# A token-mixing and two-layer network kernel: the first tokens split earlier, two weight units finished later, values loaded in longer runs

## The chip, the cores and the metric

The kernel runs on one core of a Trainium2 chip. The metric is the device time of one execution in microseconds; three executions of the kernel before were timed, and one more was recorded by the profiler. TensorE (PE) multiplies matrices, VectorE (DVE), ScalarE (ACT) and GpSimd (POOL) do elementwise work, SyncE (SP) issues most DMAs and POOL some.

## The reference

Three stages follow each other, on 8 batches of 576 tokens with 512 channels (8 heads of 64).

```python
def _attn_ref(q, k, v):
    q_s = exp(q - max(q, axis=-1)); q_s = q_s / (sum(q_s, axis=-1) + 1e-09)
    k_s = exp(k - max(k, axis=2));  k_s = k_s / (sum(k_s, axis=2) + 1e-09)
    kv = einsum('bhsd,bhse->bhde', k_s, v)
    return einsum('bhsd,bhde->bhse', q_s, kv)

def _moe_ref(x, w_tok1, w_tok2, w_ch1, w_ch2):       # w_ch1 512x1536
    h = maximum(x.T(per batch) @ w_tok1, 0.0) @ w_tok2
    u = x + h.T(per batch)
    return u + maximum(u @ w_ch1, 0.0) @ w_ch2

def _moe2_ref(x, g_ln, w_ch1, w_ch2):                # w_ch1 512x2048
    xn = (x - mean) / sqrt(var + 1e-06) * g_ln
    return x + maximum(xn @ w_ch1, 0.0) @ w_ch2
```

## The kernel before

**Attention and token mixing** run over the 8 batches, one `step(i, later)` each on every engine (`batches`). SP loads for the next batch keys, queries, values (`load_k`, `load_q`, `load_v`, L289) and transposed keys (`load_kT`), and stores the result u to DRAM. Every value product on PE (`product_kv`, L1155) multiplies the exponentials of the keys with a tile `vt` that has, for each group of 128 channels, 128 columns of values and one column of ones, whose product is the denominator. `vt` holds 5 token chunks (four of 128 rows, one of 64); one DMA per chunk fills four pieces of 128 floats (512 bytes) in each row. PE waits for all of them (`v_in`). The query side is a chain: maximum on DVE, subtraction on POOL, exponential on ACT, sum and normalisation on DVE, rounding to f32r on ACT (`hi_q`), the remainder on POOL (`lo_q`, L464), whose last part (for the 64-row chunk) is q_hi<-qt and is needed by the product at L1187.

**Precision.** Every product is made of three f32r products: high by high, high by low, low by high (`three`, L1131 to L1133). So each operand is split into a hi part (a cast on ACT) and a lo part (a subtraction on DVE or POOL).

**The two network stages** (B and C) run over tokens in passes of 924 tokens (two halves of 462; the last of a stage 912), five passes a stage. A product of 2x2 blocks is made of seven products of sums of blocks, with the sums formed on the fly. For each pass there are three (B) or four (C) mixing calls (`c.j >= 0`), each with seven products p = 0 to 6, one entry of the weight ring each, and then one finishing call with seven products of several entries (21 in B). An entry is 512 KB in DRAM, loaded by SP into a ring of four (`load_entry`), and it gives PE twelve matmuls. The ring's load n waits until PE is done with entry n - 4.

- `hi_x(pos, p)` (ACT, L566), `lo_x(pos, p)` (DVE, L834) and `sum_x(pos, i)` (DVE, L816 to L828) make the seven split operands of a pass from `xn`. For pass 0 they stand in the last batch's step and behind it: hi_x 0 and 1 in the step, 2 and 3 behind `hi_unit(6)`, 4 to 6 behind the takes of call 0.
- `take(c, p)` (ACT L650, DVE L950) moves a product from PSUM; PE's product p waits for the take of p - 2. `relu(c, p)` is L656.
- `load_x(1, c)` on SP (L328) loads the next pass; its first waits for all seven x_lo of pass 0, and stands in SP's program between ring loads.

**Weight units.** The combined, split weights of the seven products are prepared in the kernel itself, in 28 units (0 to 11 for B, 12 to 27 for C), and stored to a scratch in DRAM from which the ring reads. A unit is: two loads into `w_op` (`load_unit`, L416, L417, POOL's queue), four sums on POOL (`sum_unit`, L423 to L428), the hi part on ACT (`hi_unit`, L550), the lo part in two pieces (`lo_unit`: L434 on POOL or L841 on DVE, signal `wp_lo`), and a store of 1,792 KB (`store_unit`, L447, POOL's queue). `w_op` and `w_out` have two places; load n waits for lo n - 2. Units 0 to 7 are made beside the batches with lo on POOL; units 8 on have hi and lo at positions of the entry order (`HI_AT`), ACT's hi behind the entry's take, DVE's two halves one and two products later. The finishing call's first entries need units: its entry e (e21 + e in the count of ring entries from 0) needs units up to 7 + 2e stored, so e21 needs 0 to 7, e22 up to 9, e23 up to 11.

All orders are written out by hand; each engine runs its program in order and waits on semaphores.

Of the kernel before, what the change touches and what calls it, by code (L numbers as in the profile page):

```python
# [8 lines left out]
def mixer_kernel(nc, q, k, kT, v, w_tok1, w_tok2, w1b, w2b, g_ln, w1c, w2c, out):  # L9
    fp32, f32r = mybir.dt.float32, mybir.dt.float32r  # L10
# [17 lines left out]
    U_DVE, U_ACT = NC // 2, 2 * NC - NC // 2  # L28
    CONSTS = 10


# [21 lines left out]
    for pos in range(NX):  # L53
        stage, sg = "BC"[pos // NSG], pos % NSG
        for j in range(G1S[stage] + 1):
# [8 lines left out]

    UNITS_A = NB
    HI_AT = {e: UNITS_A + i for i, e in enumerate((2, 5, 8, 12, 27, 36))}
    HI_AT.update({(s + 1) * ENTRIES["B"] + e: UNITS_A + 6 + 5 * s + i
                  for s in range(3) for i, e in enumerate((0, 6, 11, 27, 36))})
# [43 lines left out]
    with ctx:  # L112
# [19 lines left out]
        with ExitStack() as u:  # L132
# [4 lines left out]
            with ExitStack() as a:  # L137
                kt = sb("kt", [P, NC, S], fp32, a)
                vt = sb("vt", [P, NT, NC, P + 1], fp32, a)
                ke = sb("ke", [P, NT, C], fp32, a)  # L140
# [134 lines left out]
        def _(sp):  # L275
# [10 lines left out]
            def load_v(b):  # L286
                wait(sp, kv_done, b)
                for t, rows in ST:
                    sp.dma_start(vt[0:rows, t, :, 0:P], v[b, t * P:t * P + rows, :].rearrange("p (c e) -> p c e", c=NC))\  # L289
                      .then_inc(v_in, 16)  # L290

# [113 lines left out]
        def _(pool):  # L405
# [70 lines left out]
            nc.gpsimd.memset(ke[tail, NT - 1, :], 0.0).then_inc(consts_made, 1)  # L476
            nc.gpsimd.memset(vt[tail, NT - 1, :, 0:P], 0.0).then_inc(consts_made, 1)
            pool.wait_ge(consts_made, CONSTS - 1)
# [9 lines left out]
            def step(i, later):  # L488
# [15 lines left out]
                if later:  # L504
                    lo_q(i + 1)
                lo_unit(i - 1)
                store_unit(i - 1)

            batches(step)
            load_unit(NB)  # L510
            sum_unit(NB - 1)
            lo_unit(NB - 1)
            store_unit(NB - 1)
            for n in range(NB, U0["C"] + UNITS["C"]):
                sum_unit(n)
                if n + 1 < U0["C"] + UNITS["C"]:
                    load_unit(n + 1)
                store_unit(n)


        @block.scalar
        def _(act):
# [49 lines left out]
            def step(i, later):  # L572
# [14 lines left out]
                else:  # L587
# [5 lines left out]
                    if later:  # L593
                        exp_k(i + 1, ST[0:1])
                    else:
                        hi_x(0, 0)
                    hi_qT(i, ST[4:])
                    act.wait_ge(g_done, 2 * i + 2)
# [10 lines left out]
                for c in range(NC):  # L609
# [6 lines left out]
                    if later:  # L616
# [6 lines left out]
                        if c >= 1:  # L623
                            hi_q(i + 1, ST[c - 1:c])
                    if later == 0 and c == 0:
                        hi_x(0, 1)
                if later:
# [64 lines left out]

            hi_unit(NB - 2)
            for p in (2, 3):
                hi_x(0, p)
            hi_unit(NB - 1)
            for c in CALLS:
                if c.j >= 0:
                    last = c.j == G1S[c.stage] - 1
                    for p in range(7):  # L700
                        if p in (0, 1, 2, 6):
                            take(c, p)
                        if c.index == 0 and p < 3:
                            hi_x(0, 4 + p)
                        if p == 4:
# [29 lines left out]
        def _(dve):  # L735
# [45 lines left out]
            def norm_kv(b):  # L781
# [3 lines left out]
                wait(dve, krec_made, b)  # L785
                halves = [bank[4][:, 0:2 * (P + 1)].rearrange("p (c e) -> p c e", c=2),
                          bank[1][:, 0:2 * (P + 1)].rearrange("p (c e) -> p c e", c=2)]
                for n, x in enumerate(halves):
                    nc.vector.tensor_scalar(k_den[:, 2 * n:2 * n + 2], x[:, :, P], EPS_SUM, None, ALU.add)\
                      .then_inc(kden_made, 1)  # L790
# [53 lines left out]
            def step(i, later):  # L844
# [12 lines left out]
                else:  # L857
# [15 lines left out]
                    if later:  # L873
                        sub_k(i + 1, ST[1:3])
                        max_q(i + 1, ST[2:3])
                for m in range(ND):
                    dve.wait_ge(rhi_made, ND * i + m + 1)
                    nc.vector.scalar_tensor_tensor(out=r_lo[:, m, :], in0=bank[(7, 2)[m]][:, :], scalar=0.0,
                                                   in1=r_hi[:, m, :], op0=ALU.max, op1=ALU.subtract)\
                      .then_inc(rlo_made, 1)  # L880
                if first:
                    max_q(1, ST[3:])
                    sub_k(1, ST[0:3])
                elif later:
                    max_q(i + 1, ST[3:])
                for c in range(NC):
                    if later:
# [19 lines left out]
                    if later == 0 and c == 0:  # L907
                        inputs_over(dve)
                        lo_x(0, 0)
                if later == 0:  # L910
                    lo_x(0, 1)
                    sum_x(0, 1)
                    lo_x(0, 2)
                    sum_x(0, 2)
                    lo_x(0, 3)
                    lo_x(0, 4)
                    lo_x(0, 5)
                    sum_x(0, 3)
                    lo_x(0, 6)
# [206 lines left out]
        def _(pe):  # L1126
# [17 lines left out]
            def product_kv(b):  # L1144

                pe.wait_ge(v_in, 16 * NT * (b + 1))
                wait(pe, kv_made, KV_PARTS * b)
                for c in range(NC):
# [3 lines left out]
                    for t, rows in ST:  # L1152
                        if c == 0:
                            wait(pe, kexp_made, NT * b + t + 1)
                        x = mm(dst, ke[:, t, c * P:(c + 1) * P], vt[:, t, c, :],  # L1155
                               start=t == 0, stop=t == NT - 1)
# [203 lines left out]
```

## Time and profile before

| | us |
|---|---|
| median of 3 runs | 1567.18 |
| lowest and highest | 1562.39, 1567.74 |
| the profiled execution | 1563.69 |
| its span, first to last instruction | 1561.9 |
| mean granted TensorE clock | 0.990 |

| engine | busy us | share |
|---|---|---|
| PE | 1472.2 | 94% |
| DVE | 1076.6 | 69% |
| ACT | 698.2 | 45% |
| POOL | 309.0 | 20% |

The page gives these totals, the busy shares in forty slices, the groups of instructions and the DMA issues. The attention part ends near 243 us of the span; the other views are asked for stretches: who waited for whom, an engine's instructions in order of time, and busy time, granted clock and DMA rate of a window. Times in them are microseconds from the span's start.

### The profile page before, as it was taken

To read this page: it belongs to the slowest core of one execution; us is meant where nothing else is said; L and a number is where in the kernel's file an instruction comes from. 1 tells how busy PE (TensorE), PEld (TensorE's weight loads), DVE (VectorE), ACT (ScalarE), POOL (GpSimd) and SP (SyncE) were. 2 spreads that over 40 slices of the span, in tenths; PEclk is the share of its full clock that TensorE was granted. 3 is DMA by queue.
4 is the path that set the end of the run, shared out by engine and by line. 5 is a ranking of instruction groups with operands and counts; after the bars stand their busy time and mean duration, and the time that the engine had idled before them with its cause. 6 is when DMAs were issued, how large, how long until landed. Compare 5 with 4: busy or idle time off the path is not lost.

```text
span 1561.9 us, 19837 instructions
## 1 busy us (share of the span) xinstructions
PE 1472.2 (94%) x7584; PEld 1322.4 (85%) x7584; DVE 1076.6 (69%) x1165; ACT 698.2 (45%) x844; POOL 309.0 (20%) x315
## 2 busy tenths in 40 slices
PE   6999896898999999899989999999999999999998
PEld 5988885787888887788878888888888888889998
DVE  7987876397486486496696687568657856872276
ACT  5656654352453453352452453344345424532342
POOL 6587785323303312300000000000000000000000
PEclk9999998899999999999999999999999999999999
DMA  7899985989989989979658767766876687667766
GB/s 241 256 306 296 299 282 202 403 318 366 354 291 379 372 294 362 352 288 317 240 184 300 248 209 266 249 247 219 275 243 228 237 277 244 211 219 256 251 214 199
DMA packets 150334, 429.28 MB, mean 275 GB/s; under 512 B 14240, under 2 KB 43488, under 8 KB 150240
## 3 DMA queue, kind: packets, MB, share of 16 engines
q1 hardware_dynamic: 132768, 361.94, 67.6%
q0 software_dynamic: 17472, 66.07, 11.8%
q8 instruction: 61, 1.00, 0.3%
q14 instruction: 33, 0.27, 0.1%
HBM read 348.26 MB, written 79.69 MB: 274 GB/s over the span
## 4 chain that ended last, share of the span: by engine, by line
PE 74%; DMA 10%; DVE 7%; issue 3%; SPq 2%; POOL 2%; ACT 2%; DVEq 0%; ACTq 0%; POOLq 0%
PE ps L1131 24%; PE ps L1133 23%; PE ps L1132 23%; DMA w_ring<-w_scratch_B 6%; DMA vt<-v 2%; SPq L289 2%; DMA qt<-q 1%; DVE o_lo L980 1%; DVE x_lo L834 1%; PE ps L1155 1%; DMA w_op<-w2b 1%; PE ps L1166 1%; DVE q_sum L761 1%; POOL q_lo L464 0%; DVE h L950 0%
## 5 line engine op out<-in xcount | busy, mean ns | idle before, releaser
L1131 PE MATMUL ps<-x_hi,w_ring 128*128 128x462 f32 (+1 forms) x980 | 369.2, 377 | 44.1 <-issue 15.1
L1131 PE MATMUL ps<-o_hi,w_ring 128*128 128x462 f32 (+1 forms) x980 | 367.4, 375 | 9.6 <-DVE o_lo L980 7.9
L1133 PE MATMUL ps<-x_hi,w_ring 128*128 128x462 f32 (+1 forms) x980 | 366.7, 374 | 0.0
L1132 PE MATMUL ps<-x_lo,w_ring 128*128 128x462 f32 (+1 forms) x980 | 366.7, 374 | 0.0
L1132 PE MATMUL ps<-o_lo,w_ring 128*128 128x462 f32 (+1 forms) x980 | 364.8, 372 | 0.0
L1133 PE MATMUL ps<-o_hi,w_ring 128*128 128x462 f32 (+1 forms) x980 | 364.6, 372 | 0.0
L671 ACT CAST o_hi<-h 128x924 fp32r<-128x924 f32 (+1 forms) x210 | 202.3, 963 | 254.8 <-PE ps L1133 225.0
L980 DVE TENSOR_TENSOR o_lo<-h,o_hi 128x924 fp32r<-128x924 f32 (+1 forms) x210 | 240.8, 1150 | 61.2 <-ACT o_hi L671 61.2
L1131 PEld LDWEIGHTS ps<-x_hi,w_ring 128*128 128x128 f32 x980 | 186.2, 190 | 74.3 <-issue 31.2
L1131 PEld LDWEIGHTS ps<-o_hi,w_ring 128*128 128x128 f32 x980 | 185.1, 189 | 40.1 <-issue 17.5
L950 DVE TENSOR_TENSOR h<-ps,h 128x924 f32<-128x924 f32 (+1 forms) x90 | 100.6, 1117 | 163.5 <-PE ps L1133 163.1
L1132 PEld LDWEIGHTS ps<-x_lo,w_ring 128*128 128x128 f32 x980 | 186.8, 191 | 20.6
L1133 PEld LDWEIGHTS ps<-x_hi,w_ring 128*128 128x128 f32 x980 | 186.0, 190 | 20.6
L1133 PEld LDWEIGHTS ps<-o_hi,w_ring 128*128 128x128 f32 x980 | 185.0, 189 | 20.6
L1132 PEld LDWEIGHTS ps<-o_lo,w_ring 128*128 128x128 f32 x980 | 185.1, 189 | 20.0
L650 ACT ACTIVATE h<-ps 128x924 f32<-128x924 f32 (+1 forms) x120 | 112.8, 940 | 194.9 <-PE ps L1133 194.9
L656 ACT ACTIVATE h<-h 128x924 f32<-128x924 f32 (+1 forms) x60 | 58.5, 976 | 188.3 <-DVE h L950 188.3
L992 DVE TENSOR_TENSOR res<-ps,res 128x924 f32<-128x924 f32 (+1 forms) x70 | 78.1, 1115 | 54.1 <-PE ps L1133 54.1
L834 DVE TENSOR_TENSOR x_lo<-xn,x_hi 128x924 fp32r<-128x924 f32 (+1 forms) x70 | 80.9, 1166 | 32.3 <-ACT x_hi L566 32.1
L566 ACT CAST x_hi<-xn 128x924 fp32r<-128x924 f32 (+1 forms) x70 | 66.3, 957 | 17.5 <-DVE xn L820 8.1
L671 ACT CAST o_hi<-last_pair 128x924 fp32r<-128x924 f32 (+1 forms) x35 | 33.8, 965 | 45.3 <-PE ps L1133 45.3
L980 DVE TENSOR_TENSOR o_lo<-last_pair,o_hi 128x924 fp32r<-128x924 f32 (+1 forms) x35 | 39.2, 1119 | 15.5 <-ACT o_hi L671 15.5
(140 smaller groups left out, 1831.3 us busy)
## 6 DMA issues: line engine op xcount, KB each, us to landing
w_ring<-w_scratch_C SPq DMA_DIRECT2D x280, 512.0 KB, 3.8
w_ring<-w_scratch_B SPq DMA_DIRECT2D x210, 512.0 KB, 5.6
w_scratch_C<-w_out POOLq DMA_DIRECT2D x8, 1792.0 KB, 11.7
w_scratch_C<-last_pair POOLq DMA_DIRECT2D x8, 1792.0 KB, 11.8
w_scratch_B<-w_out POOLq DMA_DIRECT2D x6, 1792.0 KB, 10.4
w_scratch_B<-last_pair POOLq DMA_DIRECT2D x6, 1792.0 KB, 9.9
kt<-kT SPq DMA_DIRECT2D x32, 288.0 KB, 6.0
u_scratch<-u_out SPq DMA_DIRECT2D x32, 288.0 KB, 3.8
```

Source lines behind the costliest of these rows:

```text
L289: sp.dma_start(vt[0:rows, t, :, 0:P], v[b, t * P:t * P + rows, :].rearrange("p (c e) -> p c e", c=NC))\
L566: nc.scalar.copy(x_hi[:, p, :, 0:n], x).then_inc(x_hi_made, 1)
L650: nc.scalar.activation(hidden(dst, c.j, c.n), bank[:, :, 0:c.n], func)\
L656: nc.scalar.activation(x, x, ACT.Relu).then_inc(relu_made, 1)
L671: nc.scalar.copy(o_hi[:, g % RO, :, 0:c.n], hidden((0, 1, 1, 2, 0, 3, 3)[p], e, c.n)).then_inc(o_hi_made, 1)
L834: nc.vector.tensor_tensor(x_lo[:, p, :, 0:n], x, x_hi[:, p, :, 0:n], ALU.subtract)\
L950: nc.vector.tensor_tensor(x, bank[:, :, 0:c.n], x, ALU.add).then_inc(taken["dve"], 1)
L980: nc.vector.tensor_tensor(o_lo[:, g % RO, :, 0:c.n], src, o_hi[:, g % RO, :, 0:c.n], ALU.subtract)\
L992: nc.vector.tensor_tensor(y, bank[:, :, 0:c.n], y, ALU.add).then_inc(taken["dve"], 1)
L1131: mm(dst, a_hi, b_hi, start=start, stop=False, skip_group_check=onto)
L1132: mm(dst, a_hi, b_lo, start=False, stop=False, skip_group_check=onto)
L1133: return mm(dst, a_lo, b_hi, start=False, stop=stop, skip_group_check=onto)
```

## The change

- `HI_AT` and `UNITS_A`: units 6 and 7 get their hi (ACT) and lo (DVE, in place of POOL) in call 0, at entries 2 and 4; units 8 to 11 move from entries 2, 5, 8, 12 to 7, 9, 12, 14; 12 and 13 stay at 27 and 36.
- POOL's loop from unit 6 on: load n + 2, store n, sums of n + 2, where it was sums of n, load n + 1, store n.
- First tokens: hi_x 1 stands directly behind hi_x 0, 2 and 3 behind the second copy of u, 4 behind the third, 5 and 6 behind the step. On DVE lo_x 0 and 1 stand ahead of r_lo, sum_x 1 behind it, lo_x 2 and sum_x 2 behind the first copy of u.
- Values: `vt` holds for each pair of channel groups 128 values, one column of ones, 128 values. The host lays v out so that a partition's rows lie one behind the other; one DMA of seven runs of 256 floats per partition, two of one run of 128 floats, and two for the 64-row chunk. The product of the second group of a pair reads from the column of ones on, so its denominator is the first column of its result.

```diff
-    UNITS_A = NB
-    HI_AT = {e: UNITS_A + i for i, e in enumerate((2, 5, 8, 12, 27, 36))}
-    HI_AT.update({(s + 1) * ENTRIES["B"] + e: UNITS_A + 6 + 5 * s + i
+    UNITS_A = NB - 2
+    HI_AT = {e: UNITS_A + i for i, e in enumerate((2, 4, 7, 9, 12, 14, 27, 36))}
+    HI_AT.update({(s + 1) * ENTRIES["B"] + e: UNITS_A + 8 + 5 * s + i
...
-                vt = sb("vt", [P, NT, NC, P + 1], fp32, a)
+                vt = sb("vt", [P, NT, NC // 2, 2 * P + 1], fp32, a)
...
-                for t, rows in ST:
-                    sp.dma_start(vt[0:rows, t, :, 0:P], v[b, t * P:t * P + rows, :].rearrange("p (c e) -> p c e", c=NC))\
-                      .then_inc(v_in, 16)
+                full = vt[:, 0:NT - 1, :, :].rearrange("p t a w -> p (t a w)")
+                w, n = 2 * P + 1, (NT - 1) * NC // 2
+                src = v[b, 0:P * n * 2 * P].rearrange("(p x) -> p x", p=P)
+                sp.dma_start(full[:, P + 1:P + 1 + (n - 1) * w].rearrange("p (n w) -> p n w", w=w)[:, :, 0:2 * P],
+                             src[:, P:P + (n - 1) * 2 * P].rearrange("p (n w) -> p n w", w=2 * P)).then_inc(v_in, 16)
+                sp.dma_start(full[:, 0:P], src[:, 0:P]).then_inc(v_in, 16)
+                sp.dma_start(full[:, n * w - P:n * w], src[:, (2 * n - 1) * P:2 * n * P]).then_inc(v_in, 16)
+                rows = ST[-1][1]
+                src = v[b, P * n * 2 * P:S * C].rearrange("(p a w) -> p a w", p=rows, w=2 * P)
+                sp.dma_start(vt[0:rows, NT - 1, :, 0:P], src[:, :, 0:P]).then_inc(v_in, 16)
+                sp.dma_start(vt[0:rows, NT - 1, :, P + 1:w], src[:, :, P:2 * P]).then_inc(v_in, 16)
...
                 if later:
                     lo_q(i + 1)
-                lo_unit(i - 1)
-                store_unit(i - 1)
+                    lo_unit(i - 1)
+                    store_unit(i - 1)
 
             batches(step)
-            load_unit(NB)
-            sum_unit(NB - 1)
-            lo_unit(NB - 1)
-            store_unit(NB - 1)
-            for n in range(NB, U0["C"] + UNITS["C"]):
-                sum_unit(n)
-                if n + 1 < U0["C"] + UNITS["C"]:
-                    load_unit(n + 1)
+            sum_unit(UNITS_A + 1)
+            for n in range(UNITS_A, U0["C"] + UNITS["C"]):
+                if n + 2 < U0["C"] + UNITS["C"]:
+                    load_unit(n + 2)
                 store_unit(n)
+                if n + 2 < U0["C"] + UNITS["C"]:
+                    sum_unit(n + 2)
...
                     else:
                         hi_x(0, 0)
+                        hi_x(0, 1)
...
-                    if later == 0 and c == 0:
-                        hi_x(0, 1)
+                    if later == 0 and c == 1:
+                        hi_x(0, 2)
+                        hi_x(0, 3)
+                    if later == 0 and c == 2:
+                        hi_x(0, 4)
...
-            hi_unit(NB - 2)
-            for p in (2, 3):
+            for p in (5, 6):
                 hi_x(0, p)
-            hi_unit(NB - 1)
...
-                        if c.index == 0 and p < 3:
-                            hi_x(0, 4 + p)
...
+                if later == 0:
+                    inputs_over(dve)
+                    lo_x(0, 0)
+                    lo_x(0, 1)
                 for m in range(ND):
                     dve.wait_ge(rhi_made, ND * i + m + 1)
...
+                if later == 0:
+                    sum_x(0, 1)
...
                     if later == 0 and c == 0:
-                        inputs_over(dve)
-                        lo_x(0, 0)
+                        lo_x(0, 2)
+                        sum_x(0, 2)
                 if later == 0:
-                    lo_x(0, 1)
-                    sum_x(0, 1)
-                    lo_x(0, 2)
-                    sum_x(0, 2)
                     lo_x(0, 3)
...
-                        x = mm(dst, ke[:, t, c * P:(c + 1) * P], vt[:, t, c, :],
+                        x = mm(dst, ke[:, t, c * P:(c + 1) * P], vt[:, t, c // 2, c % 2 * P:c % 2 * P + P + 1],
```

## Rows read from the trace of the kernel before

**Rows 1.** PE's waits, 243 to 420 us: in total, times, longest.

```profile
PE ps L1131 <- ACT h L650: 15.0, 3, 10.2
PE ps L1131 <- issue: 11.6, 3, 7.8
```

**Rows 2.** PE in order of time: start, duration, instruction, idle before it.

```profile
246.07 0.37 PE L1131 MATMUL ps<-x_hi,w_ring 128*128 128x462 f32 x1
...
258.95 0.75 PE L1131 MATMUL ps<-x_hi,w_ring 128*128 128x462 f32 x1 [10.18 <-ACT h L650]
...
263.10 0.37 PE L1131 MATMUL ps<-x_hi,w_ring 128*128 128x462 f32 x1
...
265.61 0.37 PE L1131 MATMUL ps<-x_hi,w_ring 128*128 128x462 f32 x1
...
276.11 0.72 PE L1131 MATMUL ps<-x_hi,w_ring 128*128 128x462 f32 x1 [7.82 <-issue]
...
332.94 0.37 PE L1131 MATMUL ps<-o_hi,w_ring 128*128 128x462 f32 x1
```

**Rows 3.** ACT in order of time, the first hole.

```profile
256.37 1.68 ACT L550 CAST last_pair<-w_op 128x1792 fp32r<-128x1792 f32 x1 [8.92 <-POOL w_op L428]
257.96 0.93 ACT L650 ACTIVATE h<-ps 128x924 f32<-128x924 f32 x1
```

**Rows 4.** SP's waits, 230 to 330 us.

```profile
SPq L328 <- DVE x_lo L834: 22.9, 1, 22.9
...
SPq L358 <- DMA w_scratch_B<-last_pair: 3.7, 1, 3.7
```

**Rows 5.** POOL in order of time, units 8 to 11.

```profile
266.67 1.50 POOL L428 TENSOR_TENSOR w_op<-w_op 128x256 f32<-128x256 f32 x1
...
274.16 0.96 POOL L447 DMA_DIRECT2D w_scratch_B<-w_out  x1 [4.72 <-DVE w_out L841]
...
278.72 0.58 POOL L417 DMA_DIRECT2D w_op<-w2b  x1
...
313.56 0.98 POOL L447 DMA_DIRECT2D w_scratch_B<-last_pair  x1 [5.58 <-issue]
```

**Rows 6.** DVE in order of time, one x_lo.

```profile
251.74 1.11 DVE L834 TENSOR_TENSOR x_lo<-xn,x_hi 128x924 fp32r<-128x924 f32 x1
```

**Rows 7.** Instructions that touch w_op, 0 to 330 us: ns min/median/max.

```profile
L428 POOL TENSOR_TENSOR w_op<-w_op x13: 722/737/1503, 69.8 to 319.0; 128x256 f32<-128x256 f32 x13
...
L841 DVE TENSOR_TENSOR w_out<-w_op,w_out x4: 951/1085/1226, 270.8 to 299.0; 128x1024 fp32r<-128x1024 f32 x2, 128x768 fp32r<-128x768 f32 x2
...
DMA to landing us min/median/max: 4.3/7.8/13.3
```

**Rows 8.** The page's DMA issues: count, KB each, median us to landing.

```profile
w_ring<-w_scratch_B SPq DMA_DIRECT2D x210, 512.0 KB, 5.6
...
w_scratch_B<-last_pair POOLq DMA_DIRECT2D x6, 1792.0 KB, 9.9
```

**Rows 9.** Windows: us; busy PE, PEld, DVE, ACT, POOL; clock, DMA share, GB/s.

```profile
244.00:270.00 26.00, 14.10 (x59) 11.89 (x57) 15.39 (x10) 11.85 (x12) 21.06 (x18) 0.80 0.55 193
270.00:326.00 56.00, 43.80 (x185) 37.77 (x186) 27.48 (x26) 22.35 (x23) 21.95 (x28) 0.88 1.02 392
```

**Rows 10.** DMA view, 95 to 102 us: packets by size, and SP's queue.

```profile
DMA packets 2597, 2.03 MB, mean 290 GB/s; under 512 B 132, under 2 KB 2221, under 8 KB 2596
...
q1 hardware_dynamic: 2531, 1.83, 104.0%
```

**Rows 11.** PE's waits, 0 to 330 us: in total, times, longest.

```profile
PE ps L1155 <- DMA vt<-v: 9.2, 5, 2.6
...
PE ps L1187 <- POOL q_hi L464: 2.4, 4, 0.7
```

**Rows 12.** POOL and PE in order of time, batch 3: end of q_lo, first use.

```profile
107.31 1.26 POOL L464 TENSOR_TENSOR q_hi<-qt,q_hi 64x512 fp32r<-64x512 f32 x1
...
110.59 0.28 PE L1187 MATMUL ps<-t_lo,q_hi 128*128 128x256 f32 x1
```

More of the change, by code:

```diff
@@ L29, in mixer_kernel @@
     CONSTS = 10
+    V_LOADS = 5
     SIZES = [462, 462, 462, 462, 456]
@@ L476, in _ @@
             nc.gpsimd.memset(ke[tail, NT - 1, :], 0.0).then_inc(consts_made, 1)
-            nc.gpsimd.memset(vt[tail, NT - 1, :, 0:P], 0.0).then_inc(consts_made, 1)
+            nc.gpsimd.memset(vt[tail, NT - 1, :, :], 0.0).then_inc(consts_made, 1)
             pool.wait_ge(consts_made, CONSTS - 1)
@@ L785, in norm_kv @@
                 wait(dve, krec_made, b)
-                halves = [bank[4][:, 0:2 * (P + 1)].rearrange("p (c e) -> p c e", c=2),
-                          bank[1][:, 0:2 * (P + 1)].rearrange("p (c e) -> p c e", c=2)]
+                halves = [bank[4][:, 0:2 * (P + 2)].rearrange("p (c e) -> p c e", c=2),
+                          bank[1][:, 0:2 * (P + 2)].rearrange("p (c e) -> p c e", c=2)]
                 for n, x in enumerate(halves):
-                    nc.vector.tensor_scalar(k_den[:, 2 * n:2 * n + 2], x[:, :, P], EPS_SUM, None, ALU.add)\
+                    nc.vector.tensor_scalar(k_den[:, 2 * n:2 * n + 2], bank[(4, 1)[n]][:, P:P + 2], EPS_SUM, None, ALU.add)\
                       .then_inc(kden_made, 1)
@@ L1144, in product_kv @@
             def product_kv(b):
-                pe.wait_ge(v_in, 16 * NT * (b + 1))
+                pe.wait_ge(v_in, 16 * V_LOADS * (b + 1))
                 wait(pe, kv_made, KV_PARTS * b)
@@ L1339, in tokens_first @@
         return np.ascontiguousarray(a.transpose(0, 2, 1, 3)).reshape(B, S, C)
+    values = tokens_first(inputs["v"])
+    full = values[:, 0:S // 128 * 128]
     arrays = {
@@ L1344 @@
         "kT": np.ascontiguousarray(inputs["k"].transpose(0, 1, 3, 2)).reshape(B, C, S),
-        "v": tokens_first(inputs["v"]),
+        "v": np.concatenate([full.reshape(B, -1, 128, C).transpose(0, 2, 1, 3).reshape(B, -1),
+                             values[:, S // 128 * 128:].reshape(B, -1)], axis=1),
         "w_tok1": np.ascontiguousarray(inputs["moe_w_tok1"]),
```

## The prediction

> **What bounds the kernel now.** I read the page first (TensorE, PE, is busy nearly everywhere, so only places where it stands still can give time), then PE's waits. From the end of the attention part on, three waits on ACT's `take` (h L650) hold 15.0 us and three on "issue" 11.6 us, most of it between 244 and 315 us [rows 1]. PE's own timeline then shows where. Number the entries of the weight ring e0, e1, ...; call 0 is e0 to e6, call 1 e7 to e13, call 2 e14 to e20, and the first finishing call starts at e21. e1 starts at 246.07, so e0 at 243.5 and e1 ends at 248.6; e2 starts only at 258.95; e5 at 276.11; e23 at 332.94 [rows 2]. An entry at full clock takes 265.61 - 263.10 = 2.53 us, so 23 entries are 58.2 us and took 89.4: 31 us are lost. An entry after a long stall takes 263.10 - 258.95 = 4.15 us, 1.6 more (its first product is 0.75 us long) [rows 2].
>
> ACT's timeline explains the first hole: `hi_unit(7)` (L550, last_pair) stands ahead of the first `take` and waits 8.92 us for POOL, so `take` runs at 257.96 [rows 3]. SyncE's waits explain the second: SP stands 22.9 us in `load_x(1, 0)` until the last x_lo of pass 0, and the load of e5 is queued behind it [rows 4]. A chain runs under both, the preparation of the weight units 8 to 11: load, four sums on POOL, hi on ACT, lo on DVE, store. The sums of unit 8 end at 268.17 (266.67 + 1.50), the load of unit 10 is issued at 278.72, 4.6 us after the 1,792 KB store of unit 8 (274.16), and store 11 goes out at 313.56 [rows 5]. e23 can be loaded only when that store has landed; SP waits 3.7 us for it [rows 4]. So this stretch has two clocks: PE's entries, and this chain.
>
> **The change, part by part.** Times are on the profiled run's axis, up to e23.
>
> *First tokens.* On ACT and DVE seven hi_x, seven lo_x and four sums exist before and after; some go into idle times of the last batch. x_lo costs 1.11 us [rows 6]. Following the order written out: hi_x 0 and 1 run at 229 to 231, lo_x 0 and 1 at 232.3 to 234.5 (PE's g_done is the gate), r_lo still ends at 235.9 as before, hi_x 2 and 3 at 239.6 to 241.4, hi_x 4 near 243.5, the last ACT copies of u at 245, hi_x 5 at 246, hi_x 6 at 249, behind the chain lo_x 5, sum 3 on DVE. The copies of u gate e1, wanted at 246.07: not late. `take(0,0)` follows hi_x 6, so e2 starts near 250.3 instead of 258.95: 1.7 us of stall in place of 10.3. The cover of moving hi_x 1 ahead of ACT's qT_hi 4 is about 0.3 us thin; if gone it costs 0.3. The last x_lo ends near 250.4, so `load_x(1, 0)` and then e5 are issued by 251, seven microseconds before e5 is wanted at 257.9: the 22.9 us wait and the second hole go.
>
> *Units 6 and 7.* POOL no longer makes their lo parts (two instructions each on POOL, whose stores go with them); DVE does, in halves of 1.1 us [rows 7], behind its `take`. hi 6 now sits on ACT behind e2's take, hi 7 behind e4's. What is queued behind each: on ACT the next takes, on DVE `take(0,4)`, on POOL load 8, store 6. lo 6 ends at p = 4, near 259.6. This is the step that costs: load 8 and store 6 wait for DVE there and are issued from 260 on. A load of a unit takes 4.3 us at the least, 7.8 in the middle, 13.3 at most [rows 7]; with no store ahead I take 5. Four sums of 0.74 us [rows 7] end at 268.6: equal to the 268.17 of before [rows 5]. So PE starts eight microseconds earlier and the unit chain does not start earlier.
>
> *The chain in its new order* (`load_unit(n+2)`, `store_unit(n)`, `sum_unit(n+2)`). The load now goes ahead of the store and a whole cycle behind the last one; before, load 10 stood behind store 8. But the store of unit n waits on POOL for the sums of n+1, and store 11 for those of 12. One cycle is 0.75 (first load issue) + landing + 0.15 + 2.95 (sums). The landing is the unknown: 4.3 at the low end gives 8.2, 7.8 gives 11.7, and the 13.3 of a load behind a store 17.2. I take 6, since the last store is nine microseconds old (it takes 9.9 to land [rows 8]) where the 7.8 is from loads with younger stores ahead: 10 us a cycle. Sums of 9, 10, 11, 12 end at 278.6, 288.7, 298.7, 308.8. On PE: hi 8 holds `take(1,1)` until 271.2 (0.7 stall), hi 9 holds DVE's lo 9 and `take(1,4)` until 282.6 (3.8), hi 11 holds `take(2,1)` until 302.2 (7.5, and 1.6 of clock). Store 11 goes out at 310.2, lands 9.9 to 12 us later (320.7), e23's load 5.6 after that [rows 8]: e23 starts at 326.2, seven microseconds late and again at the low clock, e24 at 326.2 + 4.15 = 330.4, where before it started at 332.94 + 2.53 = 335.5. So this region gives 5.1 us: the two holes of 18 us are filled, and most of it is given back at e13, e17 and e23.
>
> A cross-check from the DMA windows. From 244 to 270 the core moved 193 GB/s x 26 us = 5.0 MB; from 270 to 326 it was full at 392 GB/s [rows 9]. After the change entries, x loads, load 8 and store 6 make about 9.8 MB by 270. The 4.8 MB ahead are worth 12 us at 392 GB/s: the ceiling of this region's gain. With the chain as above the rest moves at about 360 GB/s, possible but near the limit.
>
> *Values in longer runs.* Bytes are the same; per batch 2,304 runs of 512 B become 896 of 1,024 and 512 of 512, in five DMAs either way. In 95 to 102 us, nearly all values, 2,221 of 2,597 packets are small and 2.03 MB take 7 us at a q1 share of 104% [rows 10]. Less the large part at 392 GB/s [rows 9] (0.96 MB, 2.45 us) that leaves 4.55 x 16 / 2,089 = 35 ns for 512 B, where 512 x 16 / 392 GB/s gives 21 ns at full rate. A 1,024 B run lies between 42 and 70 ns: 0 to 1.6 us of 16 engines saved per batch, I take 0.8. PE waits for values 9.2 us in five batches, at most 2.6, and in four it waits, at most 0.7, for POOL's q_hi [rows 11]. What is late next is this q_lo tail: in batch 3 POOL ends it at 108.57 and PE wants it at 110.59 [rows 12], 2.0 us of room. By the same two lines the other batches with a wait have 0.2 or none. So values can give at most 2.0 + 4 x 0.2 = 2.8 us unless the tail moves too; I take 2.0. Below nothing: one DMA of 896 KB might land later than four, by no more than the 0.8 saved.
> The Trainium skill (DMA: Bandwidth & Descriptors, Specifications) puts the smallest transfer for line rate at 512 B. By that rule this edit would give 0 instead of 2.0; the 35 against 21 ns speak against it.
>
> *Edits at nothing:* the memsets (POOL, before PE's first product), the reshaped k_den reads (same count), the odd chunk's moving operand at column 128 (129 columns as before), the host's reordering. Units 8 to 13 at entries 7, 9, 12, 14, 27, 36: their waits are in the chain above. Behind e24 nothing is changed but the loop order, with long POOL idle times.
>
> **Sum.** 5.1 + 2.0 = 7.1 us. The profiled run took 1563.69 us, so 1556.6. It lies 3.5 us below the median of 1567.18 (two of the three runs are near 1567.5); against the median the same gain gives 1560, which I put down.
>
> **Rivals.**
> A. The DMA lead is kept: landings of 4.5 us, cycles of 8.4, sums of 12 at 302, e24 near 324, gain 11 to 12 in the region, 13.5 in all: 1553.5. For it: queues are emptier when load 8 goes out; against it: five stores, five unit loads and ten entries, some 18 MB, still pass between 270 and e23.
> B. The unit chain gets slower and is the bound, on the slower side. Its place is POOL's `sum_unit(n+2)`, which blocks store n+1, and ACT's and DVE's hi and lo, which block the takes. e24 = end of sums 12 + 21.6; it equals 335.5 at a cycle of 11.3 us, so from a landing of 7.5 us on the region loses. With landings of 9.7 (full queues as in rows 9) cycles are 13.5, sums of 12 end at 322.6, e24 at 344: 8.7 lost, 2.0 gained, 1574.
> C. The change doesn't do what it says where it counts: values still late (0), the region near nothing (cycle 11): e24 at 334.2, gain 1.3 to 3: 1565.
> D. The q_lo tail moves along with earlier values and all 9.2 us go: 5.1 + 9.2, 1553. Against it: DVE is filled up to that tail.
>
> **Chances.** Forecast 0.45 (1557 to 1563), A 0.15, B 0.12, C 0.22, D 0.06. The range leaves out the far ends of A or D and of B: 1551 to 1570. A gain of 0.5% (7.8 us, about what a measurement here can tell from none) is below 1559.3: A, D and 0.19 of the forecast make 0.40 faster; most of B, 0.09, slower; 0.51 the same.
>
> **What would show it.** Right: e2 near 250, no wait of SP in `load_x(1, 0)` over a few us, sums 8 still ending near 268, new PE waits on take(1,4), take(2,1) and on e23's load, store 11 issued only behind sums 12. Values: the wait in batch 3 nearly gone, q_hi waits in its place elsewhere. Wrong: sums 8 well before 266, unit landings outside 5 to 7.5 us, or periods of the batches shorter by over half a microsecond each.

## The result

| | before | after |
|---|---|---|
| median of 9 runs, us | 1563.86 | 1572.59 |
| lowest to highest | 1560.21 to 1568.58 | 1568.47 to 1579.16 |
| profiled execution | 1563.69 | 1579.16 |

The ratio is 1.0058, 95% interval 1.0037 to 1.0078: the change makes the kernel 0.6% slower, where 0.5% faster was forecast and the range ended at 1570. The profiled execution of after is the slowest of its nine, so its last digits are not to be trusted. The same kernel follows below as after_again, whose profile is one of its fast executions: 1568.84 against a median of 1575.05. The profiled 1563.69 of before is a fast one too, since the medians of before on the four chips of the experiments are 1567.2 to 1568.8.

In after, `take` and `relu` on ACT are L663 and L669, PE's first product L1142, `hi_unit` L559, POOL's store L458, SP's ring load `load_entry` (L369 in its waits). PE's waits, 243 to 420 us (in total, times, longest), to be held against [rows 1]:

```profile
PE ps L1142 <- ACT h L663: 20.5, 4, 10.0
PE ps L1142 <- DMA w_ring<-w_scratch_B: 6.4, 5, 4.6
```

PE in order of time, the entries e2, e10, e17, e23 (start, duration, instruction, idle before), against [rows 2]:

```profile
249.97 0.48 PE L1142 MATMUL ps<-x_hi,w_ring 128*128 128x462 f32 x1 [1.44 <-ACT h L663]
...
278.48 0.76 PE L1142 MATMUL ps<-x_hi,w_ring 128*128 128x462 f32 x1 [8.04 <-ACT h L663]
...
311.60 0.75 PE L1142 MATMUL ps<-x_hi,w_ring 128*128 128x462 f32 x1 [9.97 <-ACT h L663]
...
334.38 0.75 PE L1142 MATMUL ps<-o_hi,w_ring 128*128 128x462 f32 x1 [4.62 <-DMA w_ring<-w_scratch_B]
```

e2 starts at 249.97 where it started at 258.95 [rows 2]; the hole at e5 is gone. At e9 PE is 20.8 us ahead of before. Then 8.0 us are lost at e10, 10.0 at e17, 4.6 at e23, and e24, at 339.2, is 3.7 us behind. SP's waits, 230 to 350 us, against [rows 4]: `load_x` waits 2.8 us in place of 22.9, the load of e23 10.7 in place of 3.7.

```profile
SPq L369 <- DMA w_scratch_B<-last_pair: 10.7, 1, 10.7
SPq L339 <- DVE x_lo L843: 2.8, 1, 2.8
```

What holds the takes at e10 and e17 is ACT's hi. ACT in order of time, hi of units 8, 9 and 11 (hi 10 began at 295.42), against [rows 3]:

```profile
275.90 1.68 ACT L559 CAST w_out<-w_op 128x1792 fp32r<-128x1792 f32 x1 [9.52 <-DMA w_scratch_B<-w_out]
...
285.17 1.69 ACT L559 CAST last_pair<-w_op 128x1792 fp32r<-128x1792 f32 x1 [5.92 <-DMA w_scratch_B<-last_pair]
...
308.17 1.68 ACT L559 CAST last_pair<-w_op 128x1792 fp32r<-128x1792 f32 x1 [9.38 <-DMA w_scratch_B<-last_pair]
```

Each begins when a store has landed, and not at once when its sums end: `hi_unit(n)` writes `w_out` at the place that unit n - 2 still occupies, and waits for that store (`wp_stored`). Behind the end of the sums this wait is worth 5.3 us for hi 8, 2.8 for hi 9, 3.3 for hi 10 and 4.2 for hi 11. POOL in order of time, last sum of 8, store 7, last sum of 11, first and last sum of 12, store 11, against [rows 5]:

```profile
269.89 0.73 POOL L439 TENSOR_TENSOR w_op<-w_op 128x256 f32<-128x256 f32 x1
...
271.87 0.98 POOL L458 DMA_DIRECT2D w_scratch_B<-last_pair  x1
...
303.20 0.72 POOL L439 TENSOR_TENSOR w_op<-w_op 128x256 f32<-128x256 f32 x1
...
311.02 1.71 POOL L434 TENSOR_TENSOR w_op<-w_op 128x256 f32<-128x256 f32 x1 [4.72 <-DMA w_op<-w1c]
...
315.78 1.50 POOL L439 TENSOR_TENSOR w_op<-w_op 128x256 f32<-128x256 f32 x1
...
318.70 0.97 POOL L458 DMA_DIRECT2D w_scratch_B<-last_pair  x1
```

Here POOL itself waits only for its unit loads: none of its loads and stores between 268 and 319 us shows an idle time before it, so the lo parts that they need were ready. The late hi parts hold PE at e10 and e17, but neither the sums of 12 nor store 11 waits for them. Whether lo 11, which DVE makes at 309.9 to 313.6 and so partly beside the sums of 12, slows those sums more than its other work does, no run separates.

The DMA windows, against [rows 9]: the lead is made (293 GB/s in place of 193 in the first window), then lost (346 in place of 392), while PE's busy time in the second falls from 43.8 to 34.9 us.

```profile
244.00:270.00 26.00, 24.56 (x117) 21.69 (x116) 13.66 (x14) 12.21 (x14) 4.49 (x7) 1.00 0.81 293
270.00:326.00 56.00, 34.87 (x142) 29.10 (x141) 27.42 (x24) 22.64 (x23) 31.05 (x35) 0.85 0.90 346
```

And the values: PE's waits, 0 to 243 us, against [rows 11]. The wait for values shrinks by 3.2 us, the one for POOL's q_hi grows by 2.1.

```profile
PE ps L1166 <- DMA vt<-v: 6.0, 5, 1.9
PE ps L1198 <- POOL q_hi L475: 4.5, 5, 1.6
```

### The profile page after: what moved, and what is told of

The parts are those of the page before. It is cut to its first block, busy times and chain, and to the rows that moved or that the text cites. A ratio compares the mean times of both kernels' runs of the same rounds, so it can differ in the third digit from the quotient of the medians.

```text
span 1577.4 us, 19837 instructions
## 1 busy us (share of the span) xinstructions
PE 1480.1 (94%) x7584; PEld 1326.7 (84%) x7584; DVE 1069.5 (68%) x1169; ACT 698.2 (44%) x844; POOL 303.6 (19%) x311
## 3 DMA queue, kind: packets, MB, share of 16 engines
q0 software_dynamic: 17472, 66.07, 11.5%
## 4 chain that ended last, share of the span: by engine, by line
PE 70%; DMA 15%; DVE 8%; issue 3%; POOL 3%; SPq 1%; ACT 1%; DVEq 0%; ACTq 0%; POOLq 0%
PE ps L1142 23%; PE ps L1144 22%; PE ps L1143 22%; DMA w_ring<-w_scratch_B 9%; DMA qt<-q 2%; DMA w_op<-w2b 2%; DVE x_lo L843 1%; DMA vt<-v 1%; DVE q_sum L770 1%; POOL q_lo L475 1%; DMA w_scratch_B<-last_pair 1%; DVE qt L787 1%; DVE o_lo L991 1%; PE ps L1177 1%; DVE q_den L778 1%
## 5 line engine op out<-in xcount | busy, mean ns | idle before, releaser
L1142 PE MATMUL ps<-x_hi,w_ring 128*128 128x462 f32 (+1 forms) x980 | 370.8, 378 | 45.5 <-ACT h L663 20.5
L1142 PE MATMUL ps<-o_hi,w_ring 128*128 128x462 f32 (+1 forms) x980 | 368.1, 376 | 16.9 <-DMA w_ring<-w_scratch_B 9.9
L991 DVE TENSOR_TENSOR o_lo<-h,o_hi 128x924 fp32r<-128x924 f32 (+1 forms) x210 | 237.1, 1131 | 63.8 <-ACT o_hi L684 63.8
L1142 PEld LDWEIGHTS ps<-x_hi,w_ring 128*128 128x128 f32 x980 | 187.3, 191 | 76.1 <-issue 25.1
L1142 PEld LDWEIGHTS ps<-o_hi,w_ring 128*128 128x128 f32 x980 | 185.6, 189 | 48.1 <-issue 13.9
L663 ACT ACTIVATE h<-ps 128x924 f32<-128x924 f32 (+1 forms) x120 | 112.4, 940 | 207.0 <-PE ps L1144 207.0
L1143 PEld LDWEIGHTS ps<-o_lo,w_ring 128*128 128x128 f32 x980 | 185.6, 189 | 20.4
L669 ACT ACTIVATE h<-h 128x924 f32<-128x924 f32 (+1 forms) x60 | 58.5, 976 | 172.4 <-DVE h L961 172.4
L575 ACT CAST x_hi<-xn 128x924 fp32r<-128x924 f32 (+1 forms) x70 | 66.3, 958 | 22.9 <-DVE xn L829 12.7
## 6 DMA issues: line engine op xcount, KB each, us to landing
w_scratch_C<-last_pair POOLq DMA_DIRECT2D x8, 1792.0 KB, 14.5
w_scratch_B<-w_out POOLq DMA_DIRECT2D x6, 1792.0 KB, 10.5
```

The source lines that it names most:

```text
L575: nc.scalar.copy(x_hi[:, p, :, 0:n], x).then_inc(x_hi_made, 1)
L663: nc.scalar.activation(hidden(dst, c.j, c.n), bank[:, :, 0:c.n], func)\
L669: nc.scalar.activation(x, x, ACT.Relu).then_inc(relu_made, 1)
L991: nc.vector.tensor_tensor(o_lo[:, g % RO, :, 0:c.n], src, o_hi[:, g % RO, :, 0:c.n], ALU.subtract)\
L1142: mm(dst, a_hi, b_hi, start=start, stop=False, skip_group_check=onto)
L1143: mm(dst, a_hi, b_lo, start=False, stop=False, skip_group_check=onto)
```

## The experiments

Each kernel was timed in rounds beside the kernel before on one chip, in twelve executions (hi_late eleven, before_load_first and early_apart six); four chips were used in all. The ratio is to before, with its 95% interval. "e0 to e24" and "e24 to e126" are differences of entry starts in PE's timeline of the one profiled execution (an entry is twelve products, four of them on the line that is L1131 in before, and starts with the first of these, as in [rows 2]). In before they are 91.9 and 280.9 us; in the profiled after 95.9 and 293.0. From e126 to the end all kernels take 944.0 to 948.7 us, from e210 on 718.6 to 720.4, so what differs lies ahead of that.

| kernel | ratio | interval | e0 to e24 | e24 to e126 |
|---|---|---|---|---|
| after_again | 1.0055 | 1.0031 to 1.0079 | 92.7 | 289.8 |
| v_only | 0.9994 | 0.9970 to 1.0018 | 91.3 | 286.5 |
| tokens_only | 0.9986 | 0.9964 to 1.0009 | 87.8 | 283.1 |
| units_only | 1.0064 | 1.0037 to 1.0090 | 97.8 | 288.2 |
| store_first | 0.9983 | 0.9960 to 1.0006 | 92.3 | 286.5 |
| store_first_late | 1.0008 | 0.9985 to 1.0031 | 92.8 | 283.0 |
| hi_late | 1.0065 | 1.0042 to 1.0088 | 95.0 | 289.5 |
| early | 0.9990 | 0.9971 to 1.0009 | 84.0 | 290.3 |
| before_load_first | 1.0071 | 1.0044 to 1.0099 | 90.8 | 291.5 |
| store_load_at_once | 1.0024 | 0.9998 to 1.0049 | 90.7 | 287.5 |
| load_after_landing | 0.9968 | 0.9950 to 0.9985 | 91.2 | 281.1 |
| early_late | 0.9957 | 0.9934 to 0.9980 | 82.8 | 288.7 |
| early_store_first | 0.9952 | 0.9924 to 0.9981 | 89.7 | 291.8 |
| early_store_first_2 | 0.9949 | 0.9927 to 0.9970 | 84.3 | 291.3 |
| early_apart | 0.9900 | 0.9871 to 0.9929 | 84.8 | 280.4 |

### Which part of the change costs

The three parts alone, put on the kernel before, and the whole once more.

> The kernel before with the values' new layout and five new loads alone. Theory S (the loss sits in the chain of the weight units, where ACT's hi of unit n waits until the store of unit n - 2 has landed): values do almost nothing, 0 to 2 us faster, PE's waits for values fall from 9.2 to about 6 us and those for POOL's q_hi rise from 2.4 to about 4.5. Rival V (the new loads or the tiles' new places cost time): this kernel alone is slower by 4 us or more.

> The kernel before with the new places of hi_x, lo_x and sum_x for pass 0 alone; units and values as before, hi of unit 7 still ahead of the first take. Theory S: the hole at e2 stays (8 to 11 us, it hangs on POOL's lo 6 and sums 7), the hole at e5 goes (7.8 us and 1.6 of clock), units 8 to 11 keep their chain and order, so some of it is given back at the next hi; 0 to 6 us faster in all. Rival V gives the same here. Rival T (the moved splits delay the last batch or e0): slower by 1 us or more, e0 later than 244.5.

> The kernel before with units 6 and 7 finished in call 0, units 8 to 11 at entries 7, 9, 12, 14 and the new loop order on POOL; first tokens and values as before. Theory S: all of the loss is here, 6 to 12 us slower than before: the hole at e2 goes, new holes at e10 and e17 of about 8 and 10 us, and e23 waits for store 11. Rival V: the same as before within 3 us.

> The changed kernel once more, beside the others on one chip. Its profiled run was the slowest of nine, with 3.7 us behind at e24 and 15.5 at the end. Expected: 8 to 9 us slower than before by the rounds; if the profile is of an ordinary run, e24 again 3 to 5 us behind and a smaller loss after it, by waits of single entries for their loads.

Values 0.9994 and first tokens 0.9986, both within their uncertainty of nothing; units 1.0064, the whole loss. In units_only the hole at e17 is 9.1 us and e23 waits 4.7, near what was expected; the one at e10 is 4.4 and not 8. In v_only the waits moved as theory S said: those for values lost 5.2 us (9.2 to 4.0) and those for q_hi gained 2.0 (2.4 to 4.4). In tokens_only the hole at e5 went and the one at e2 stayed, as said (e0 to e24 4.1 us shorter). after_again, 1.0055, has e0 to e24 at 92.7, next to before, and e24 to e126 at 289.8 against 280.9: there the larger loss is behind e24, in a part that I had costed at nothing. In units_only the two stretches lose nearly alike, 5.9 and 7.3 us. Single profiles scatter here (with POOL's old order and the old start of the units 280.9 to 286.5 us, with the new order 288.2 to 293.0), so the verdicts below go by the rounds and use the profiles for the place.

### POOL's order, before and behind unit 12

```diff
 # store_first (units 6 on); store_first_late has it from unit 12 on
             for n in range(UNITS_A, U0["C"] + UNITS["C"]):
-                if n + 2 < U0["C"] + UNITS["C"]:
-                    load_unit(n + 2)
                 store_unit(n)
-                if n + 2 < U0["C"] + UNITS["C"]:
-                    sum_unit(n + 2)
+                if UNITS_A < n < U0["C"] + UNITS["C"] - 1:
+                    sum_unit(n + 1)
+                if n + 2 < U0["C"] + UNITS["C"]:
+                    load_unit(n + 2)
```

> The changed kernel with POOL's order of before from unit 6 on: store n, sums of n + 1, load n + 2; all else as changed. Theory S (ACT's hi of unit n waits for the landing of store n - 2, and the new order issues each store only behind the next sums): store 7 goes out near 264 and not near 272, hi 9 and hi 11 run some 5 us earlier than in the changed kernel (285 and 308), store 11 is no longer behind sums 12, e24 comes 3 to 9 us earlier relative to e0, total 3 to 12 us faster than the changed kernel. Rival P (the places 2, 4, 7, 9, 12, 14 of hi cost it, not the order): the holes at e10 and e17 and the total stay within 2 us of the changed kernel.

> The changed kernel with POOL's order of before from unit 12 on only; units 6 to 11 in the new order. Theory L (a second loss behind e24, where a load and the 1,792 KB store of a unit go out together ahead of a pass's first entries): e0 to e24 as in the changed kernel (93 to 96 us), e24 to e126 back from 290 to 293 us to 281 to 287 us; 4 to 8 us faster than the changed kernel. Against L: e24 to e126 stays at 289 us or more, then the second loss is a consequence of what happens before e24 or is spread otherwise.

With the old order everywhere the changed kernel is at 0.9983, with it from unit 12 on at 1.0008: of the 0.7% between 1.0055 and 0.9983 about two thirds (0.5%, 7 us) come from units 12 to 27, the rest, within the intervals, from units 6 to 11. Theory S was half right in the first part. Store 7 goes out at 263.93 as expected, but hi 9 and hi 11 begin at 287.9 and 311.0, 2.8 and 2.9 us later than in after and not 5 earlier. In store_first hi 8 to 11 no longer wait for stores, but for sums, 31 us in all, because each load now stands behind a store. The holes at e10 and e17 stay, 10.4 and 8.0 us for 8.0 and 10.0, and e17 comes 71.0 us after e0 (68.3 in after). Only the wait of e23 goes. So the wait for the store, taken away, was replaced by one for the sums at once, and e24 hardly moved (92.3 against 92.7 and 95.9). ACT's waits in store_first, 240 to 345 us:

```profile
ACT w_out L559 <- POOL w_op L439: 16.0, 2, 11.9
ACT last_pair L559 <- POOL w_op L439: 15.2, 2, 8.8
```

Then the reverse: the kernel before, with only units 12 on in the new order.

```diff
 # before_load_first
+            sum_unit(12)
+            load_unit(13)
+            sum_unit(13)
+            for n in range(12, U0["C"] + UNITS["C"]):
+                if n + 2 < U0["C"] + UNITS["C"]:
+                    load_unit(n + 2)
+                store_unit(n)
+                if n + 2 < U0["C"] + UNITS["C"]:
+                    sum_unit(n + 2)
```

> The kernel before, its attention part, first tokens and units 0 to 11 untouched; from unit 12 on POOL takes the new order (load n + 2, store n, sums n + 2). Theory L (the order alone costs the time behind e24, since a unit's load goes out just ahead of its store and the store lands later): e0 to e24 as before (92 us), e24 to e126 288 to 293 us in place of 281 to 286, stores of C land in 14 us in place of 12, total 5 to 8 us slower than before. Against L: total within 2 us of before; then the second loss needs the shifted first part too.

1.0071, as much as the whole change (1.0055 to 1.0064). Ahead of e24 little differs (90.8 against 91.9), e24 to e126 takes 291.5. This one edit, in a place where POOL is idle most of the time, costs by itself what the change costs. It moves two things at once: the load of unit n + 2 goes out just ahead of store n, and the sums of n + 2 follow as soon as it lands, where before had the sums of n + 1. The sums show no cost of their own: in 345 to 630 us four of them take 4.1 us on average here and 4.2 in before, and DVE's o_lo, the most frequent of its instructions, takes 1,152 ns with the load ahead and 1,246 in before.

### The places of hi, and the start of the chain

```diff
 # hi_late, on the changed kernel
-    HI_AT = {e: UNITS_A + i for i, e in enumerate((2, 4, 7, 9, 12, 14, 27, 36))}
+    HI_AT = {e: UNITS_A + i for i, e in enumerate((2, 4, 10, 14, 17, 19, 27, 36))}
```

> The changed kernel with hi of units 8 to 11 at entries 10, 14, 17, 19 in place of 7, 9, 12, 14. Theory S (the chain load, sums, hi, lo, store of the units sets e24; the holes at e10 and e17 are only where PE meets it): the holes move to later entries and shrink, e24 stays within 3 us of the changed kernel's or comes later, since store 11 goes out no earlier; total within 3 us of the changed kernel. Rival P (the early places of hi block ACT and DVE and are themselves the cost): e24 4 us or more earlier and the total 4 us or more faster.

The holes do not shrink, they join: e17 starts 49 us after e0 in place of 68, and e23 then waits 19.2 us for its load. e0 to e24 is 95.0, as in after. So the holes at e10 and e17 are where PE meets the chain of units, not what delays e24; rival P is out. PE's waits for ring loads in hi_late, 240 to 345 us:

```profile
PE ps L1142 <- DMA w_ring<-w_scratch_B: 24.0, 6, 19.2
```

In early, units 6 and 7 are finished in idle times of the last batch's step, which starts the chain earlier.

```diff
 # early (ACT, ACT, DVE, DVE), on the changed kernel; HI_AT 4, 8, 12, 15 for units 8 to 11
+                if later == 0:
+                    hi_unit(NB - 2)          # behind r_hi
...
             hi_x(0, 5)
+            hi_unit(NB - 1)
             hi_x(0, 6)
...
                     if later == 0 and c == 0:
+                        lo_unit(NB - 2, 0)
+                        lo_unit(NB - 2, 1)
                         lo_x(0, 2)
...
                     lo_x(0, 6)
+                    lo_unit(NB - 1, 0)
+                    lo_unit(NB - 1, 1)
```

> The changed kernel with units 6 and 7 not in call 0 but earlier, in idle times of the last batch's step: hi 6 behind r_hi, lo 6 on DVE behind its first copy of u, hi 7 ahead of hi_x 6, lo 7 behind lo_x 6; units 8 to 11 at entries 4, 8, 12, 15. Theory S: the unit chain starts 15 us earlier (store 6 near 245, sums 8 near 253), the holes at e10 and e17 shrink to under 3 us each, e24 comes 8 to 15 us earlier than in the changed kernel, bounded by the DMA rate; the total is below the kernel before by 2 to 8 us. Rival B (the DMA rate alone sets e24, whatever the chain): e24 within 3 us of the changed kernel's.

> Units 6 and 7 finished in the last batch's step, units 8 to 11 in the new order, POOL's order of before from unit 12 on. Theories S and L add up: e0 to e24 84 us as in the early kernel, e24 to e126 283 to 286 us, total 7 to 12 us below the kernel before. If the DMA rate is what is left, the gain of the first part is paid back behind e24 (290 us) and the total is 2 us below before.

> The same early units 6 and 7, with POOL's order of before (store n, sums n + 1, load n + 2). Theory S and L together: the fastest of the four, 5 to 12 us below the kernel before. If only S holds, equal to the one with the new order within 3 us up to e24.

> The same kernel as early_store_first, whose one profiled execution was the slowest of its twelve, for an ordinary profile and a second set of rounds. Expected: 0.3 to 0.8% below before again; in an ordinary profile e0 to e24 84 to 90 us and e24 to e126 under 288 us.

In early the sums of 8 end 9.1 us after e0 where they end 27.3 us after it in after, and e0 to e24 falls to 84.0, 8.7 to 11.9 us less than in after, which rules out rival B. With the new order behind unit 12 the total is no better than before (0.9990), with the old one it is 0.9957, 0.9952 and 0.9949; the interval of the first overlaps two of these three and just misses the last. The order of units 6 to 11 makes no difference that these runs can tell. The gain did not come through whole. early_late has 288.7 us from e24 to e126, not the 283 to 286 expected, in an execution near its median (1561.33 against 1559.14), and its total is 0.43% or 7 us below before, the near end of the 7 to 12 expected: part of the gain ahead of e24 is paid back behind it. The profiled executions of early_store_first and early_store_first_2 were the slowest of their twelve (1571.71 and 1568.57 against medians of 1562.24 and 1558.31), so their 291 us are no measure of the kernel; the rounds are. The profile that early_store_first_2 was run for was again not an ordinary one.

### What in the new order costs

```diff
 # store_load_at_once, on the kernel before from unit 12 on
                 store_unit(n)
+                load_unit(n + 2)
                 sum_unit(n + 1)
-                load_unit(n + 2)
 # load_after_landing
                 store_unit(n)
                 sum_unit(n + 1)
+                pool.wait_ge(wp_stored[n % 2], 16 * (n // 2 + 1))
                 load_unit(n + 2)
```

> The kernel before; from unit 12 on POOL issues store n and at once load n + 2, then the sums of n + 1. Store first as before, but both transfers go out together as in the new order. If the issue at one moment costs the time (burst): as slow as before_load_first, 1.005 or more, e24 to e126 288 us or more. If the load's place ahead of the store costs it (order): within 2 us of before, stores of C land in 11 to 13 us.

> The kernel before; from unit 12 on POOL waits until store n has landed before it issues load n + 2 (units have 15 to 30 us each, so nothing waits for the load). If the overlap of the two is what costs ring loads their time (burst): 0.1 to 0.4% faster than before, e24 to e126 under 281 us, unit loads land in about 5 us. If order: the same as before within 2 us. If the total bytes set it: the same.

> early_store_first with the load of unit n + 2 behind the landing of store n from unit 12 on. If burst: 1 to 5 us faster than early_store_first (0.995 of before), 0.990 to 0.994 of before. If order or bytes: 0.995 again.

Neither pure answer holds. Store first and the load at once behind it is 1.0024, a third of the loss, with an interval (0.9998 to 1.0049) that does not quite exclude none. The load behind the store's landing is 0.9968, clearly below before and, on the same chip, clearly below at once. In before the load goes out 3.9 to 7.5 us behind the store, behind the landing 10 to 15 us. So the ratios rise from apart (0.9968) over before (1) and at once (1.0024) to load ahead (1.0071), but of the neighbours only the step from apart to before is clear of the noise. The chip of before_load_first was another than that of the two kernels of this section, each beside its own runs of before. The medians from issue to landing, 345 to 630 us, in us:

| kernel | ring load, 512 KB | unit load, 256 KB half (w2c) | unit store, 1,792 KB (w_out) |
|---|---|---|---|
| load_after_landing | 6.1 | 4.7 | 13.7 |
| before | 6.5 | 8.6 | 11.5 |
| store_load_at_once | 6.3 | 11.3 | 12.5 |
| before_load_first | 7.3 | 5.7 | 14.5 |

The ring loads' lines of before, before_load_first and load_after_landing:

```profile
w_ring<-w_scratch_B SPq DMA_DIRECT2D x104, 512.0 KB, 6.5
```

```profile
w_ring<-w_scratch_B SPq DMA_DIRECT2D x99, 512.0 KB, 7.3
```

```profile
w_ring<-w_scratch_B SPq DMA_DIRECT2D x103, 512.0 KB, 6.1
```

The ring loads, which PE waits for, follow the totals at both ends (7.3, 6.5, 6.1), the store's own landing does not; at once has 6.3, so the median alone does not rank that one. From e24 to e126 PE stands idle 15.1 us with the load behind the landing, 16.9 in before, 20.4 at once and 23.5 with the load ahead. The rest of the 10.5 us between before and before_load_first, 3.8 us, lies in entries that take longer behind such a wait, e42 and e84 above all. The profile of before has no such entry in this stretch and load_after_landing has four, 4.3 us together, which is why these two profiles do not differ (280.9 and 281.1) though the rounds do.

The waits lie at single entries, most of the longest at the first of a pass, where SP loads the next pass too and stores the last. Those at e84 and e126 grow (1.7 and 1.3 us in before, 3.0 and 3.9 with the load ahead), the one at e42 does not (3.5 and 3.0). Where POOL's load falls beside these three entries differs too. It goes out 15 to 16 us ahead of them with the load ahead, 11 to 13 at once, 5 to 11 in before, and 1.7 to 2.5 us behind their start in load_after_landing. There it is also not always apart from a store: in four of twelve units the next store follows the load within 3.1 us, in two of them as closely as with the load ahead, and this kernel is still the faster one.

```profile
410.72 0.75 POOL L416 DMA_DIRECT2D w_op<-w1c  x1 [11.01 <-DMA w_scratch_C<-w_out]
...
412.19 0.97 POOL L447 DMA_DIRECT2D w_scratch_C<-last_pair  x1
```

So two readings are left, that the two transfers cost when they are in the queues together, and that the load costs when it is there ahead of a pass's first entries. No run separates them, and what the 16 engines do with the transfers the runs do not show.

early_apart, 0.9900, is the best of all: 1% below before, 1.5% below the change. Its e0 to e24 is 84.8, its e24 to e126 280.4.

## Why the prediction was wrong

- **First tokens: right.** e2 was put at 250.3 and came at 249.97, the stall there at 1.7 and was 1.44; SP's wait fell to 2.8 us and the hole at e5 went. The part is worth less than its 18 us, since the chain takes it back: tokens_only 0.9986.
- **Load 8 at 260, sums 8 at 268.6:** load 8 was issued at 260.1, sums 8 ended at 270.6 (the load took 6.8 us to land, not 5). That the unit chain would not start earlier was the right reading, and early shows what an earlier start is worth.
- **The holes at e10 and e17: failed, by a wait left out.** The sum takes hi to begin when the sums end (268.6, 278.6, 288.7, 298.7). `hi_unit(n)` waits for store n - 2 too, which the section on the kernel does not name, and the change put each store behind the next sums: store 7 goes out at 271.87, behind sums 8, and hi 9 begins at 285.17, 13.3 us later. hi 8 to 11 came at 275.9, 285.2, 295.4 and 308.2, of which the store's wait is 5.3, 2.8, 3.3 and 4.2 us. PE's stalls on take(1,1), take(1,4) and take(2,1) were put at 0.7, 3.8 and 7.5 us and were 8.0, 1.2 and 10.0.
- **The cycle, "0.75 + landing + 0.15 + 2.95": failed, by a term mis-sized.** By the rows of POOL this term, and not the store's wait, sets e24. The landings of the unit loads were near the guess of 6 (5.4 to 7.3), but four sums took 3.8, 3.8, 4.0 and 6.3 us (the last from 311.0 to 317.3) in place of 2.95. The four cycles took 46.7 us where 40.2 stood. Sums 12 ended at 317.3, not 308.8: of these 8.5 us about 6 are slow sums, 2 the later sums 8, and the rest landings and rounding. e24 = end of sums 12 + 21.6 held: 338.9 by it, 339.2 measured. The sum was right and its input 8.5 us off. This was rival B's side (12%), with its point of decision, a cycle of 11.3 us, passed at 11.7, but not by the landings of over 7.5 us that B named.
- **"Behind e24 nothing is changed but the loop order, with long POOL idle times": failed, and the larger part.** The prediction put the new order at nothing because POOL is idle there. What it moved was the moment at which 2.3 MB enter the DMA queues beside the ring loads. before_load_first prices this alone at 0.71% (0.44 to 0.99), some 11 us; in the profiles 280.9 became 291.5. How the order costs this inside the queues stays open.
- **Values: mechanism right, size unproved.** The next late thing was the q_lo tail, as said. Of the 2.0 us nothing can be told from 0.9994 with an interval of 0.24% either way, nor of the 0 that the prediction worked out from the Trainium skill (DMA: Bandwidth & Descriptors, Specifications). e0 starts at 238.8 to 245.3 us in the eleven profiles with the new values and at 240.5 to 245.9 in the six without, 241.6 against 242.9 on average, which is inside the scatter. PE's waits for values did shrink, so they landed earlier against PE's need of them. The small packets between 95 and 102 us fell from 2,221 [rows 10] to 1,435, q1's share from 104.0% to 84.5%, in a window that holds more of POOL's queue than before (0.63 MB for 0.19). That short runs cost more per byte is neither shown nor refuted by the time.
- **The range** ended 2.6 us below the median: it took in neither the loss behind e24 nor both losses at once.

## What to carry to other kernels

When an order of DMA issues is changed, do not price it by the issuing engine's idle time, but by what else is in the queues at that moment. Read it at the entries with the least slack, and try issuing a transfer that has time only when the large one ahead of it has landed (here 0.3% alone, and 1.0% in the changed kernel with the earlier start of the chain). Before a producer is moved, list every wait of its consumer, buffer reuse among them: a hi that waits for data also waits for the store that frees its place. Price a repeated instruction by what it takes beside the engine that will be busy then, not by its median. Filling a hole in front of a chain that does not start earlier moves the hole.

## What the runs showed of the hardware

- The order and distance of a 512 KB load and a 1,792 KB store in POOL's queue changed the kernel's time by 1% between the extremes, at the same bytes: 0.9968 with the load 10 to 15 us behind the store, 1.0071 with it 1.3 to 1.9 us ahead. A half of the load landed in 4.7 us behind the landed store, in 5.7 ahead of the store, in 8.6 some 4 to 7 us behind it and in 11.3 at once behind it; the ring loads of the other queue landed in 6.1 to 7.3.
- An entry after an idle time of PE takes either 2.6 us, at a granted clock of 1.00, or 3.6 to 4.2, at 0.57 to 0.69, and the idle time before it does not tell which: 3.48 us and then 2.61 at e42 of before, 1.96 us and then 4.15 at e126 of load_after_landing. So a short wait for the ring can cost up to 1.6 us more than it shows.
- Four sums on POOL took 6.3 us beside a busy DVE (311.0 to 317.3 us of after) against 2.95 alone, and DVE's x_lo in the same microseconds took 1.65 in place of 1.11. This agrees with the Trainium skill (SBUF — State Buffer, SBUF: two separate sides): GpSimd and VectorE share a pair of ports under an exclusive lock, taken also by a DVE instruction with two SBUF inputs, and the loser waits for the whole instruction. Slow sums were in the trace of before (4.3 us for the four of unit 12), and I priced the cycle without them.
- The Trainium skill (DMA: Bandwidth & Descriptors, Queues, rings and completion order) has each engine change between queues by packets. By that, as I read it, the order within POOL's queue would not touch SP's ring loads. At once (1.0024) and load ahead (1.0071) differ in that order, but also in when the sums run and in the chip, and their intervals overlap; so the runs neither show nor refute it.
